# Two expert tiles of the first batch, routed during attention and run while the last batch is routed

## The chip, the cores and the metric

The kernel runs on one core of a Trainium2 chip. The metric is the time of one execution on the device in microseconds (us). The engines are named as the profile names them: PE is TensorE (PEld its weight loads), DVE is VectorE, ACT is ScalarE, POOL is GpSimd, SP is SyncE, whose queue issues most of the DMAs.

## What is computed

Three stages follow each other, cut here to what matters:

```python
def attention(q, k, v):                    # 4 batches, 8 heads, 768 rows, 64 wide
    scores = q @ k.T / 8                   # kept: the first 4 keys, and the last 128 up to the row
    return softmax(scores) @ v
x = attention(...)                         # as 3072 rows of 512
logits = x @ w_gate + modality_bias[modality_id]      # 8 experts
e = argmax(logits); gate = softmax(logits)[e]
moe[rows of e] = gate * (relu(x[rows] @ w1[e]) @ w2[e])   # w1 512x1024, w2 1024x512
h = moe @ w_in                             # 512x2048
out = (h * sigmoid(1.702 * h)) @ w_out     # 2048x512
```

Every row goes to one expert only. All of it is float32. The wide products are made from a rounded part (hi) and the rest (lo) of each operand as hi*hi + hi*lo + lo*hi in the type fp32r, so each operand is "split": one pass rounds it (ScalarE or GpSimd), another subtracts (VectorE or GpSimd).

## The kernel before

**Attention** goes over 4 batches of 8 heads of 6 row blocks (48 steps for a batch, `each_step`). At step n TensorE makes the scores of block n (lines 753, 754), turns the probabilities of block n-3 (line 765) and weighs the values of block n-4 (line 790). VectorE masks scores (line 1396), ScalarE makes the exponentials (line 1054) and copies turned probabilities out of PSUM (line 1079; VectorE does so for a head's last block, line 1408). All engines run their steps in program order, so what is put in a step holds up what stands behind it. After a head VectorE divides it by its row sums into `x_sb` (at step 4 of the next head). GpSimd splits q and k of the heads (lines 578 to 587); the arrays have four slots, so it may start head g only when head g-4's scores are made.

SyncE's queue works pair by pair (two heads, g from 0 to 15). For each pair it waits for `heads_done` of both heads, stores their part of x to DRAM (line 400), loads vT for pair g+3 (line 388), then v and q, k of the next batch (lines 377, 379, 372), and at last 256 KB of the second layer's input weights `w_in` into `win_raw` (line 395).

**Routing.** The logits of the heads are made inside attention. Batches 0 to 2 are routed during batch 3's attention (GpSimd and VectorE, `route_early`). The last batch is routed behind attention: argmax on VectorE, ranks by small matmuls (lines 864 to 870), positions, a sort of tokens into tiles of 128 rows by 24 one-hot matmuls (line 880), then the same for the gates (line 888). Between these, TensorE runs filler matmuls (`keep_going`, line 854). The first expert's weights are loaded (line 459, four pieces of 1 MB) when the ranks are known.

**The expert loop** takes a tile of 128 rows of one expert: GpSimd gathers rows by an indirect DMA (line 680), TensorE turns them (line 899), ScalarE rounds (line 1125), VectorE subtracts (line 1593), TensorE multiplies by w1 (lines 914 to 916, 24 matmuls), ScalarE applies relu (line 1132), TensorE turns the result (line 926) and multiplies by w2 (lines 939 to 941, 24 matmuls); VectorE scales by the gate (line 1608), GpSimd scatters the rows to `y_rows` (line 689). GpSimd splits `win_raw` among the first four tiles (lines 661, 663). The loop's length and each tile's expert are read from a table made by the routing. Then the dense second layer follows (lines 973 to 984).

Of the kernel before, what the change touches and what calls it, by code (L numbers as in the profile page):

```python
# [22 lines left out]
P = 128  # L23
BANK = 512
F32 = mybir.dt.float32
# [12 lines left out]
DMA = 16  # L38


def program(nc, qkT, vT, vP, modality, w_gate, bias, w1, w2, w_in, w_out, out, n_sink, window):
# [18 lines left out]
    EXP_AT, RANK_AT_STEP = 41, 41  # L60
    WARM_UP = 7
    CH = DM // P
# [4 lines left out]
    LEAD = 4  # L67
    YW = DM + 1
# [55 lines left out]
    with ExitStack() as ctx:  # L124
# [52 lines left out]
        q_st = place("q_st", [P, SLOT, S], F32R, at=ZW)  # L177
        k_hi = place("k_hi", [P, SLOT, KEYS], F32R)
        k_lo = place("k_lo", [P, SLOT, KEYS], F32R)
        v_sb = place("v_sb", [P, PAIRS, QT, VPAIR])  # L180
        x_sb = place("x_sb", [P, QT, DM])
        assert top[0] <= ZW + 2 * HALVES
        qk_raw = place("qk_raw", [P, SLOT, 2, S], at=ZS)
# [60 lines left out]
        table_f = place("table_f", [P, TAB])  # L244
        s_msk = place("s_msk", [P, RING, WMAX])
        assert top[0] <= ZS

# [3 lines left out]
        oh_slot = place("oh_slot", [P, NTILE, P], F32R, at=ZW + 2 * HALVES)  # L251
        tile_eq = place("tile_eq", [P, NTILE, SLOTS])
        tile_tok = place("tile_tok", [P, NTILE, SLOTS], F32R)
        assert top[0] <= ZW + 2 * HALVES + CH * F2
# [5 lines left out]
        GATES_AT = top[0]  # L260
# [3 lines left out]
        assert top[0] <= ZS  # L264
        tile_gate = place("tile_gate", [P, NTILE, 2, SLOTS], F32R, at=GATES_AT)
# [50 lines left out]
        expert_known, consts_copied = sem("expert_known"), sem("consts_copied")  # L316
        ohs_ready = sem("ohs_ready")
# [43 lines left out]
        TURN_AFTER = {5 + 2 * t: t for t in range(GT)}  # L361

# [4 lines left out]
        def _(sp):  # L367
# [55 lines left out]
            for h in range(SLOT + 1, H):  # L423

                sp.wait_ge(qk_split, 3 * (h - SLOT))
                load_qk(0, h)
                if h == SLOT + 1:
                    load_vt(2)
            for b in range(B):
                for c in range(PAIRS):  # L430
# [32 lines left out]
            load_win(B * PAIRS - 1)  # L463
            sp.wait_ge(runs_ready, 1)
            total = sp.value_load(table[0:1, TOTAL:TOTAL + 1], min_val=NTILE - 4, max_val=SLOTS - 4) + 4
# [13 lines left out]
            def rows_of(g):  # L479

                tiles = (g + 1) * GT + GT + E
# [33 lines left out]
        def _(pool):  # L515
# [74 lines left out]
            for h in range(1, B * H):  # L590
                split_qk(*divmod(h, SLOT))

            full, some = [P, NTILE, E], [P, PRE, E]
# [4 lines left out]
            pool.wait_ge(consts_loaded, 32)  # L598
            then(pool.tensor_copy(mod_f[:], mod_i[:, :, 0]))
            for m in range(NM):  # L600
                then(pool.tensor_scalar(mod_eq[:], mod_f[:], float(m), None, ALU.is_equal))
                to = bias_of[:] if m == 0 else biases[:]
                then(pool.tensor_tensor(to, col(mod_eq[:], full), bias_sb[:, m:m + 1, :].broadcast_to(full), ALU.mult))
                if m:
                    then(pool.tensor_tensor(bias_of[:], bias_of[:], biases[:], ALU.add))
            pool.wait_ge(logits_added, B - 1)
            pool.tensor_tensor(lg[:, 0:PRE, :], lg[:, 0:PRE, :], bias_of[:, 0:PRE, :], ALU.add).then_inc(pre_biased, 1)

            pool.wait_ge(best_found, 1)
# [6 lines left out]
                .then_inc(ties_marked, 1)  # L616

# [9 lines left out]
            then(pool.tensor_copy(acc[:, 1], hot[:, 0]))  # L627
            for t in range(1, QT - 1):
                then(pool.tensor_tensor(acc[:, t + 1], acc[:, t].bitcast(F32), hot[:, t], ALU.add))
# [10 lines left out]
            pool.wait_ge(rows_known, 1)  # L640
            for t in range(PRE):
                pool.tensor_scalar(oh_slot[:, t, :], iota_row[:], rank_p[:, t:t + 1], None, ALU.is_equal)\
                    .then_inc(rows_marked, 1)

# [1087 lines left out]
```

## Time and profile before

| | us |
|---|---|
| median of 3 runs | 1115.92 (1115.02 to 1116.5) |
| the profiled execution | 1115.81 |
| its span | 1113.9 |
| TensorE busy | 1101.5 (99%) |
| VectorE, ScalarE, GpSimd busy | 424.2, 378.1, 327.0 |
| mean granted TensorE clock | 0.997 of 2.4 GHz |

The span goes from the first to the last instruction of the profiled execution. A busy TensorE is one with matmuls in flight; they overlap, so starts matter more than durations. In the span attention takes about the first 234 us, the last batch's routing goes on to about 262, the expert loop to about 585 and the second layer to the end. A row in order of time gives the start and the duration in us, the engine, the line, the operation with its output and inputs, the shapes, how many were merged, and in brackets how long the engine had been idle before it and what ended that. A row of groups gives count, busy us, mean ns of one, and the idle time before.

### The profile page before, as it was taken

The numbers are of one execution on the slowest core, as the hardware profiler recorded it, in microseconds if no ns is written. First come the engines' busy times: TensorE is split into PE (matmuls) and PEld (weight loads), VectorE is DVE, ScalarE is ACT, GpSimd is POOL, SyncE is SP. The second block draws the span as 40 slices with busy tenths as digits, with TensorE's granted clock in tenths as the row PEclk, the third lists the DMA queues.
The fourth block names the chain that finished last, engine by engine and source line by source line (L and its number), as shares of the span: only waits on it lengthen the run. The fifth ranks groups of instructions, "written<-read, shape, count | busy, mean of one in ns | idle before, by whom it ended". The sixth has DMA issues, their size and how long they took to land.

```text
span 1113.9 us, 18738 instructions
## 1 busy us (share of the span) xinstructions
PE 1101.5 (99%) x5952; PEld 943.1 (85%) x5953; DVE 424.2 (38%) x1089; ACT 378.1 (34%) x781; POOL 327.0 (29%) x441
## 2 busy tenths in 40 slices
PE   9999999999999999999999999999999999999998
PEld 8999999987888888888888888888888888888887
DVE  5566666685121233221265323222322222222222
ACT  3666666643221233222253222222222222222222
POOL 8898888644642212121121001001001001000100
PEclk9999999989999999999999999999999999999999
DMA  9999988237111123211132101001000000000101
GB/s 222 234 259 243 229 223 222 73 124 264 38 47 47 41 99 139 79 47 38 38 125 103 29 1 48 19 9 38 28 9 38 19 19 28 9 0 0 39 1 38
DMA packets 57393, 92.04 MB, mean 83 GB/s; under 512 B 7937, under 2 KB 32769, under 8 KB 57345
## 3 DMA queue, kind: packets, MB, share of 16 engines
q1 hardware_dynamic: 51584, 72.56, 24.2%
q0 software_dynamic: 5760, 18.89, 4.9%
q8 instruction: 24, 0.39, 0.2%
q14 instruction: 25, 0.20, 0.1%
HBM read 72.02 MB, written 19.41 MB: 82 GB/s over the span
## 4 chain that ended last, share of the span: by engine, by line
PE 92%; DVE 3%; ACT 2%; issue 2%; POOL 1%; ACTq 0%; DVEq 0%; POOLq 0%
PE psum L982 8%; PE psum L984 8%; PE psum L983 8%; PE psum L975 8%; PE psum L973 8%; PE psum L974 8%; PE psum L790 5%; PE psum L939 4%; PE psum L914 4%; PE psum L941 4%; PE psum L916 4%; PE psum L915 4%; PE psum L940 4%; PE psum L765 2%; PE psum L926 2%; PE psum L753 2%
## 5 line engine op out<-in xcount | busy, mean ns | idle before, releaser
L1654 DVE TENSOR_TENSOR g<-psum,g 128x512 f32<-128x512 f32 x96 | 66.3, 691 | 292.3 <-ACT g L1178 292.3
L1178 ACT ACTIVATE g<-psum 128x512 f32<-128x512 f32 x96 | 57.3, 598 | 306.5 <-PE psum L975 305.7
L982 PE MATMUL psum<-w_hi,gT_hi 128*128 128x512 f32 x384 | 151.3, 394 | 0.0
L984 PE MATMUL psum<-w_hi,gT_lo 128*128 128x512 f32 x384 | 149.6, 390 | 0.0
L983 PE MATMUL psum<-w_lo,gT_hi 128*128 128x512 f32 x384 | 149.6, 389 | 0.0
L975 PE MATMUL psum<-x2T,win_lo 128*128 (+1 forms) x384 | 149.5, 389 | 0.0
L973 PE MATMUL psum<-x2T,win_hi 128*128 (+1 forms) x384 | 149.5, 389 | 0.0
L974 PE MATMUL psum<-x2T,win_hi 128*128 (+1 forms) x384 | 149.4, 389 | 0.0
L722 POOL DMA_INDIRECT out<-o_out,out_rows x20 | 21.5, 1075 | 406.6 <-ACT o_out L1198 402.0
L790 PE MATMUL psum<-v_sb,pT 128*128 128x73 f32 x704 | 106.0, 269 | 2.4 <-DVE pT L1408 1.2
L1396 DVE CUSTOM_DVE_ANT_0 s_msk<-psum,mask_sb 128x260 f32<-128x260 f32 (+1 forms) x192 | 75.0, 403 | 70.7 <-PE psum L754 37.5
L790 PEld LDWEIGHTS psum<-v_sb,pT 128*128 128x128 f32 x704 | 93.4, 191 | 8.9 <-DVE pT L1408 7.5
L1054 ACT ACTIVATE probs<-s_msk,negmax 128x260 f32<-128x260 f32 (+1 forms) x192 | 93.5, 494 | 13.8 <-DVE negmax L1396 13.6
L1661 DVE TENSOR_TENSOR gT_lo<-g,gT_hi 128x512 fp32r<-128x512 f32 x96 | 66.4, 693 | 64.5 <-ACT gT_hi L1185 64.5
L914 PE MATMUL psum<-w_hi,xsT_hi 128*128 128x512 f32 x208 | 83.3, 400 | 2.0 <-DVE xsT_lo L1593 2.0
L984 PEld LDWEIGHTS psum<-w_hi,gT_lo 128*128 128x128 f32 x384 | 72.1, 188 | 15.3
L975 PEld LDWEIGHTS psum<-x2T,win_lo 128*128 128x128 f32 x384 | 72.1, 188 | 15.0
L974 PEld LDWEIGHTS psum<-x2T,win_hi 128*128 128x128 f32 x384 | 72.1, 188 | 15.0
L1185 ACT CAST gT_hi<-g 128x512 fp32r<-128x512 f32 x96 | 59.6, 621 | 74.1 <-DVE g L1654 74.1
L973 PEld LDWEIGHTS psum<-x2T,win_hi 128*128 128x128 f32 x384 | 72.1, 188 | 14.9
L983 PEld LDWEIGHTS psum<-w_lo,gT_hi 128*128 128x128 f32 x384 | 72.2, 188 | 14.4
L982 PEld LDWEIGHTS psum<-w_hi,gT_hi 128*128 128x128 f32 x384 | 72.1, 188 | 14.3
(229 smaller groups left out, 1991.4 us busy)
## 6 DMA issues: line engine op xcount, KB each, us to landing
qk_raw<-qkT SPq DMA_DIRECT2D x64, 384.0 KB, 7.6
stage<-w SPq DMA_DIRECT2D x12, 1024.0 KB, 6.9
x<-y_rows SPq DMA_DIRECT2D x24, 256.5 KB, 2.6
vT_sb<-vT SPq DMA_DIRECT2D x16, 384.0 KB, 6.0
v_sb<-vP SPq DMA_DIRECT2D x16, 384.0 KB
x_rows<-x_sb SPq DMA_DIRECT2D x16, 384.0 KB, 3.2
win_raw<-w_in SPq DMA_DIRECT2D x16, 256.0 KB, 8.7
stage<-w_out SPq DMA_DIRECT2D x4, 1024.0 KB, 6.6
```

The costliest lines, as they stand in the source:

```text
L790: mm = pe.matmul(o, pT[:, n % 2, k * P:(k + 1) * P], v_sb[:, c, kb, half * VEXT:(half + 1) * VEXT], start=(i == 0 and k == 0), stop=(k == ...
L914: pe.matmul(psum[:, HB[hf], :], xsT_hi[:, c, :], hi, start=(c == 0), stop=False)
L973: pe.matmul(bank, wh, hi, start=(c == 0), stop=False)
L974: pe.matmul(bank, wh, lo, start=False, stop=False)
L975: mm = pe.matmul(bank, win_lo[:, c, f * P:(f + 1) * P], hi, start=False, stop=(c == CH - 1))
L982: pe.matmul(psum[:, OB[t], :], gh, hi, start=(f == 0), stop=False)
L983: pe.matmul(psum[:, OB[t], :], gh, lo, start=False, stop=False)
L984: return pe.matmul(psum[:, OB[t], :], gT_lo[:, f % 4, t * P:(t + 1) * P], hi, start=False, stop=(f == F2C - 1))
L1054: act.activation(probs[:, n % RING, 0:width[i]], s_msk[:, n % RING, 0:width[i]], ACT.Exp, bias=negmax[:, n % 8:n % 8 + 1], scale=-1.0).the ...
L1396: dve.tensor_tensor_reduce(s_msk[:, n % RING, 0:width[i]], psum[:, S_ps[n % 3], 0:width[i]], mask_sb[:, min(i, MASKS - 1), 0:width[i]], -S ...
L1654: dve.tensor_tensor(g32[:, f % 2, :], psum[:, FB[f % 2], :], g32[:, f % 2, :], ALU.mult)\
L1661: dve.tensor_tensor(gT_lo[:, f % 4, :], g32[:, f % 2, :], gT_hi[:, f % 4, :].bitcast(F32), ALU.subtract).then_inc(gT_split, 1)
```

## The change

Two tiles ("open" tiles, `OPEN = 2`) are filled with the first batch's rows of the expert that most of them choose, up to 256 rows.

- Batch 0 is routed by itself during batch 1: GpSimd makes logits, ties, one-hots and running counts between its head splits (`between`, behind heads 9, 11, 12, 13, 17, 18, 25), VectorE the reductions in steps 9 to 46 of batch 1, TensorE the ranks at step 29. In step 42 VectorE waits for GpSimd (`open_chosen`). In batch 2 a sort gives tokens and gates of the two tiles. The rows taken are subtracted from the expert's ranks, so that the loop does not hold them.
- SyncE loads that expert's w1 and w2 in 16 parts of 128x512 (256 KB), two with each pair from pair 7 to 14, behind the vT load and ahead of the next batch's v, q and k. The 16 loads of `w_in` leave attention and are issued when both open tiles are done.
- ScalarE rounds part j at step 2 of head 17+j (`round_open`), GpSimd subtracts it behind the split of head 21+j, the last four behind its one-hots.
- GpSimd gathers the open rows near the end of batch 3. TensorE turns the first tile in the tail of attention.
- Behind attention TensorE runs the two open tiles' matmuls with the routing's small matmuls in between, in an order written out by hand; the filler is gone. In `up` and `down` the products of a half are grouped: all hi*hi, then hi*lo, then lo*hi, each group with its own wait. `EXP_AT`, `RANK_AT_STEP` and the steps of `route_early` move back by 1 to 5.
- Arrays are placed anew: the open tiles use the room of `win_hi` and `win_raw`; `x_sb` lies where `w_hi` is later, so ScalarE waits for the last stores of x before it rounds the first run's weights.

```diff
@@ SyncE, for each pair
                     store_pair(b, c)
                     if g + 3 < B * PAIRS:
                         load_vt(g + 3)
+                    if g == OPEN_LOAD:
+                        sp.wait_ge(open_expert_known, 1)
+                        chosen = sp.value_load(open_e[0:1, 0:1], min_val=0, max_val=E - 1)
+                    if OPEN_LOAD <= g < OPEN_LOAD + OPEN_PARTS // 2:
+                        load_open(g - OPEN_LOAD, chosen)
...
-                    if g + 1 < B * PAIRS:
-                        load_win(g)
@@ SyncE, behind attention
-                        if q == 2:
-                            sp.wait_ge(gathered, 16)
...
-            load_win(B * PAIRS - 1)
+            sp.wait_ge(y_ready, OPEN)
+            for n in range(QUARTERS * PIECES):
+                load_win(n)
@@ GpSimd
+            between = {9: make_biases, 11: open_logits, 12: open_ties, 13: open_chain, 17: open_choice,
+                       18: open_marks, 25: open_rows}
             for h in range(1, B * H):
                 split_qk(*divmod(h, SLOT))
+                if h in between:
+                    between[h]()
+                if h >= OPEN_BACK:
+                    split_open(h - OPEN_BACK)
@@ ScalarE, in each step
+                if b == 1 and n == 2 * QT + 2:
+                    act.wait_ge(open_shifted, 1)
+                    act.activation(o_exps[:], o_below[:], ACT.Exp).then_inc(open_exped, 1)
+                j = (b * HT + n - 2) // QT - OPEN_HEAD
+                if n % QT == 2 and 0 <= j < OPEN_PARTS and (n < HT or b == B - 1):
...
+                    round_open(j)
...
+            def round_open(j):
+                q, cols = open_part(j)
+                act.wait_ge(open_loaded[j // 2], 32)
+                act.copy(win_hi[:, q, cols], win_raw[:, q, cols]).then_inc(open_high, 1)
@@ TensorE, behind attention (the filler calls keep_going go)
+            for hf, part in ((0, 0), (0, 1), (1, 0)):
+                up_open(0, hf, part)
+            rank_own()
+            turn_open(1)
+            up_open(0, 1, 1)
+            turn_h(0)
+            for hf in range(2):
+                for part in range(2):
+                    up_open(1, hf, part)
+            pe.wait_ge(heads_done, B * H + AHEAD)
+            down_open(0, 0, 0)
+            sort_tokens()
+            down_open(0, 0, 1)
+            down_open(0, 1, 0)
+            down_open(0, 1, 1)
+            turn_h(1)
             turn_xs(0)
+            sort_gates()
+            down_open(1, 0, 0)
+            down_open(1, 0, 1)
             up(0, 0)
             turn_xs(1)
+            down_open(1, 1, 0)
+            down_open(1, 1, 1)
@@ VectorE, in batch 1
+                if n == 42:
+                    dve.wait_ge(open_chosen, 1)
+                    then(dve.tensor_reduce(o_row[:], o_rank[:], AX.X, ALU.add))
+                if n == 43:
+                    then(dve.tensor_reduce(o_most[:], o_which[:], AX.X, ALU.add))
+                if n == 44:
+                    dve.tensor_copy(open_e[:], o_most[:]).then_inc(open_expert_known, 1)
```

## Rows read from the trace of the kernel before

**Rows 1.** Page, costliest groups: expert up part, first of three products.
```profile
L914 PE MATMUL psum<-w_hi,xsT_hi 128*128 128x512 f32 x208 | 83.3, 400 | 2.0 <-DVE xsT_lo L1593 2.0
```

**Rows 2.** Windows, attention and gap: busy PE, PEld, DVE, ACT, POOL; clock; DMA.
```profile
160.00:200.00 40.00, 39.48 (x327) 37.34 (x325) 25.32 (x120) 25.56 (x75) 32.46 (x37) 1.00 0.89 219
244.00:252.00 8.00, 8.00 (x44) 8.00 (x45) 6.82 (x16) 3.80 (x2) 1.24 (x1) 0.57 0.57 204
```

**Rows 3.** TensorE in order of time between attention and the expert loop.
```profile
233.25 0.71 PE L795 MATMUL psum<-v_sinks,pT_sinks 128*128 128x292 f32 x2
...
236.24 0.30 PE L864 MATMUL psum<-seen,ones 128*128 128x64 f32 x1 [0.51 <-DVE onehot L1324]
...
242.62 3.34 PE L880 MATMUL psum<-tile_tok,oh_slot 128*128 128x32 f32 x24 [1.20 <-DVE tile_tok L1498]
...
256.28 0.50 PE L914 MATMUL psum<-w_hi,xsT_hi 128*128 128x512 f32 x1 [1.47 <-DVE xsT_lo L1593]
...
261.87 0.60 PE L899 MATMUL psum<-ident,xs 128*128 128x128 f32 x4
262.58 1.09 PE L926 MATMUL psum<-ident,h 128*128 128x128 f32 x8
264.20 0.49 PE L914 MATMUL psum<-w_hi,xsT_hi 128*128 128x512 f32 x1 [0.53 <-DVE xsT_lo L1593]
```

**Rows 4.** TensorE in order of time, first up matmul of two following tiles.
```profile
276.46 0.47 PE L914 MATMUL psum<-w_hi,xsT_hi 128*128 128x512 f32 x1
...
288.76 0.48 PE L914 MATMUL psum<-w_hi,xsT_hi 128*128 128x512 f32 x1
```

**Rows 5.** SyncE's issues in order of time, pairs 8 and 12.
```profile
142.54 0.40 SPq L400 DMA_DIRECT2D x_rows<-x_sb  x1
142.98 0.54 SPq L388 DMA_DIRECT2D vT_sb<-vT  x1
...
197.00 0.40 SPq L400 DMA_DIRECT2D x_rows<-x_sb  x1
...
198.03 0.73 SPq L395 DMA_DIRECT2D win_raw<-w_in  x1
```

**Rows 6.** DMA issues of pairs 8, 12: KB each, us to landing.
```profile
vT_sb<-vT SPq DMA_DIRECT2D x1, 384.0 KB, 4.3
...
vT_sb<-vT SPq DMA_DIRECT2D x1, 384.0 KB, 5.4
win_raw<-w_in SPq DMA_DIRECT2D x1, 256.0 KB, 5.4
```

**Rows 7.** ScalarE in order of time, head 19, and one pass of 128x512.
```profile
143.81 0.81 ACT L1054 ACTIVATE probs<-s_msk,negmax 128x128 f32<-128x128 f32 x2
145.28 0.27 ACT L1079 COPY pT<-psum 128x128 f32<-128x128 f32 x1 [0.67 <-PE psum L765]
...
254.85 0.59 ACT L1125 CAST xsT_hi<-psum 128x512 fp32r<-128x512 f32 x1 [4.88 <-PE psum L899]
```

**Rows 8.** TensorE in order of time, value matmuls of head 19's first block.
```profile
146.88 0.34 PE L790 MATMUL psum<-v_sb,pT 128*128 128x73 f32 x2
```

**Rows 9.** GpSimd in order of time: splits of two heads, the bias block.
```profile
53.36 0.84 POOL L578 CAST q_st<-qk_raw 128x768 fp32r<-128x768 f32 x1
...
57.10 1.82 POOL L585 TENSOR_TENSOR k_lo<-qk_raw,k_hi 128x768 fp32r<-128x768 f32 x1
...
59.04 0.83 POOL L578 CAST q_st<-qk_raw 128x768 fp32r<-128x768 f32 x1
...
207.81 0.19 POOL L599 CAST mod_f<-mod_i 128x24 f32<-128x24 int32 x1
...
210.70 0.52 POOL L607 TENSOR_TENSOR lg<-lg,bias_of 128x144 f32<-128x144 f32 x1
```

**Rows 10.** VectorE in order of time around step 42 of batch 1.
```profile
115.25 0.28 DVE L1396 CUSTOM_DVE_ANT_0 s_msk<-psum,mask_sb 128x128 f32<-128x128 f32 x1
...
117.37 0.41 DVE L1408 COPY pT<-psum 128x256 f32<-128x256 f32 x1
```

More of the change, by code:

```diff
@@ L588, in split_qk, with col, row, make_biases @@
                     .then_inc(qk_split, 1)
+            full, some, batch = [P, NTILE, E], [P, PRE, E], [P, QT, E]
+            def col(v, shape):
+                return v.rearrange("p (t o) -> p t o", o=1).broadcast_to(shape)
+            def row(v, shape):
+                return v.rearrange("p (o e) -> p o e", o=1).broadcast_to(shape)
+            def make_biases():
+                pool.wait_ge(consts_loaded, 32)
+                then(pool.tensor_copy(mod_f[:], mod_i[:, :, 0]))
+                for m in range(NM):
+                    then(pool.tensor_scalar(mod_eq[:], mod_f[:], float(m), None, ALU.is_equal))
+                    to = bias_of[:] if m == 0 else biases[:]
+                    then(pool.tensor_tensor(to, col(mod_eq[:], full), bias_sb[:, m:m + 1, :].broadcast_to(full),
+                                            ALU.mult))
+                    if m:
+                        then(pool.tensor_tensor(bias_of[:], bias_of[:], biases[:], ALU.add))
@@ new lines, in open_logits, with open_ties @@
+            def open_logits():
+                pool.wait_ge(logits_added, 1)
+                pool.tensor_tensor(o_lg[:], lg[:, 0:QT, :], bias_of[:, 0:QT, :], ALU.add).then_inc(open_biased, 1)
+            def open_ties():
+                pool.wait_ge(open_best, 1)
+                pool.tensor_tensor(o_below[:], o_lg[:], col(o_best[:], batch), ALU.subtract).then_inc(open_shifted, 1)
+                pool.wait_ge(open_shifted, 1)
+                then(pool.tensor_scalar(o_tied[:], o_below[:], 0.0, None, ALU.is_equal))
+                pool.tensor_tensor(o_tied[:], o_tied[:], row(from_end[:], batch), ALU.mult).then_inc(open_tied, 1)
@@ new lines, in open_chain @@
+            def open_chain():
+                pool.wait_ge(open_lead, 1)
+                then(pool.tensor_tensor(o_tied[:], o_tied[:], col(o_lead[:], batch), ALU.subtract))
+                then(pool.tensor_scalar(o_hot[:], o_tied[:], 0.0, None, ALU.is_equal))
+                then(pool.tensor_scalar(o_seen[:, 0, :], from_end[:], 0.0, None, ALU.mult))
+                for t in range(QT):
+                    then(pool.tensor_tensor(o_seen[:, t + 1, :], o_seen[:, t, :].bitcast(F32),
+                                            o_hot[:, t, :].bitcast(F32), ALU.add))
+                pool.sem_inc(open_seen, 1)
@@ L626, in _ @@
             acc = seen[:, 0:PRE, :].rearrange("p (b t) e -> p t b e", b=B - 1)
-            then(pool.tensor_copy(acc[:, 1], hot[:, 0]))
-            for t in range(1, QT - 1):
+            for t in range(QT - 1):
                 then(pool.tensor_tensor(acc[:, t + 1], acc[:, t].bitcast(F32), hot[:, t], ALU.add))
@@ L643, in _ @@
                     .then_inc(rows_marked, 1)
+            for j in range(B * H - OPEN_BACK + 1, OPEN_PARTS):
+                split_open(j)
             def finish_scatter():
@@ L841, in step @@
                     weigh_values(b, n - PV_LAG)
+                if b == B - 1 and n == HT + 1:
+                    turn_open(0)
             def warm_up():
@@ new lines, in down_open @@
+            def down_open(t, hf, part):
+                chunks = [(hf * FC // 2 + k, slice(k * DM, (k + 1) * DM)) for k in range(FC // 2)]
+                if part == 0:
+                    pe.wait_ge(y_moved, t + PRIMED)
+                    pe.wait_ge(hT_high, t * 2 + hf + 1)
+                    pe.wait_ge(open_high, 4 * (hf + 3))
+                    for f, cols in chunks:
+                        pe.matmul(psum[:, YB, :], hT_hi[:, f, :], win_hi[:, 2 + hf, cols], start=(f == 0), stop=False)
+                else:
+                    pe.wait_ge(open_split, 4 * (hf + 3))
+                    for f, cols in chunks:
+                        pe.matmul(psum[:, YB, :], hT_hi[:, f, :], win_lo[:, 2 + hf, cols], start=False, stop=False)
+                    pe.wait_ge(hT_split, t * 2 + (hf + 1 + H_FREE))
+                    for f, cols in chunks:
+                        mm = pe.matmul(psum[:, YB, :], hT_lo[:, f, :], win_hi[:, 2 + hf, cols],
+                                       start=False, stop=(f == FC - 1))
+                    if hf:
+                        mm.then_inc(y_ready, 1)
@@ new lines, in up @@
+                    pe.wait_ge(w1_split, r * 2 + hf + 1)
+                    for c in range(CH):
+                        pe.matmul(psum[:, HB[hf], :], xsT_hi[:, c, :], w_lo[:, hf, chunks[c]], start=False, stop=False)
+                    if hf == 0:
+                        pe.wait_ge(xsT_split, t + 1 + PRIMED)
+                    for c in range(CH):
+                        mm = pe.matmul(psum[:, HB[hf], :], xsT_lo[:, c, :], w_hi[:, hf, chunks[c]],
+                                       start=False, stop=(c == CH - 1))
```

530 lines of the change are left out of this document (379 added, 151 removed).

## The prediction, made before any run of the change

> **What bounds the kernel now.** I read the page's costliest groups, then busy time by stage, then the engines in order of time where stages meet. The 208 matmuls at line 914, eight to a tile, say that 26 expert tiles run [rows 1]. In attention TensorE is busy 39.5 of 40 us at the full clock, while GpSimd is busy 32.5 and the DMA engines 0.89 of the time [rows 2]. So in attention a delay of TensorE is not won back, and GpSimd's spare time is small. The gain has to come from the stretch behind attention. The last attention matmul ends at about 233.9 us and the expert loop's first transpose starts at 262.58 [rows 3]: 28.7 us in which much of what TensorE does is filler (line 854, dropped by the change). A tile in the loop takes 12.30 us, from 276.46 to 288.76 [rows 4].
>
> **What is removed.** In those 28.7 us the useful work is: rank matmuls 1.1 us (236.24 to about 237.3), the two sorts of 24 matmuls at 3.34 (the tokens' stands in the rows, the gates' is as long), two groups of four transposes at 0.45 (the second from 261.87), and the first tile's up part from 256.28 to 261.87, 5.6; together 14.3 [rows 3]. The other 14.4 us are filler and waits. The change puts two tiles' work, 2 x 12.3 = 24.6 us, in front and between the sorts, and takes it from the loop: with the reference's seeded inputs the first batch sends 399 rows to expert 0, so both tiles are full, and the experts' counts 1567, 1497 and 8 (13 + 12 + 1 = 26 tiles, as the trace has it) become 11 + 12 + 1. So the loop starts at 233.9 + 14.3 + 24.6 = 272.8 if TensorE never waits, and has two tiles fewer: 24.6 - (272.8 - 262.6) = 14.4 us won. The stall of 0.7 us in the old loop's first pass (transposes from 262.58 for 0.87, next matmul at 264.20 [rows 3]) goes too, as the split of the second gathered tile is done by then. Against it, the transposes of tile 0's second half are late: its relu can only start when the eight matmuls behind the ranks end, and with 0.59 us for such a ScalarE pass [rows 7] TensorE waits some 0.5 us. Net **-14.6**. Between 13 and 15.5: the token sort now ends near 252 and not 246, so the first gather is issued near 253.5 and wanted near 257.3, where it may be a microsecond late.
>
> **What is costed at nothing.** Grouping the hi and lo products of a tile leaves their number and size alone. The run weights (4 MB) still come at the routing's end, but are now wanted at 264 us, not at 256. The second layer's input weights leave attention and load after both open tiles, hidden by 24 loop tiles. On GpSimd a head's split takes 5.68 us [rows 9] of TensorE's 6.8 per head; from head 21 on each also carries the split of a 128x512 part, two thirds of the 1.82 that 768 elements take [rows 9], so 1.2: 6.9 in all. It no longer gains on TensorE, but it doesn't collapse, as it may run 15 us behind (it works three heads ahead) and I count 8. If that cover went, every microsecond beyond would be TensorE's.
>
> **A wait of VectorE, step 42 of batch 1.** It waits there for GpSimd's choice. GpSimd, which starts head 9's split at 59.04 [rows 9], then does the bias block (207.81 to 210.70, 2.9 us, moved here [rows 9]), eight heads at 5.68, and 17 small operations at about 0.3, so it is done at 59.0 + 5.7 + 2.9 + 45.4 + 5.3 = 118.3. VectorE is at the wait at 115.6 (mask at 115.25 [rows 10]). Queued behind it is the copy of turned probabilities at 117.37 [rows 10], and it comes 2.9 late; I give TensorE 0.4 of slack before it wants the copy. **+2.5**, between 0 (GpSimd on time) and 4.
>
> **A wait of ScalarE, eight times.** This term decides. SyncE issues part pair k of the expert's weights (2 x 256 KB) behind the store of x and the load of vT of pair 7+k, and that store waits for step 4 of head 16+2k. ScalarE rounds the first of them at step 2 of head 17+2k, four steps later, in order, with the exponentials and copies of probabilities queued behind. Take T as the store's issue, 142.54 for pair 8, 0.44 ahead of vT's [rows 5]. ScalarE ends the exponential before that place at 144.62, T+2.1; the next copy is at 145.28 [rows 7]; TensorE starts the matmuls on it at 146.88, T+4.34 [rows 8]. When do the parts land? The vT load, issued at 142.98, landed 4.3 us later, T+4.7 [rows 5, 6], and the parts are behind it. With pair 12, vT (issued 0.45 behind its store, too) landed at T+5.9 and one more piece of 256 KB, issued at 198.03, 5.4 later, T+6.4 [rows 5, 6]. So a piece adds 0.6, or 1.1 by what the full DMA engines move in attention (219 GB/s at 0.89 [rows 2]). Two pieces give T+5.9 to 6.9 from pair 8, T+7.0 to 7.5 from pair 12; I take T+6.7. Then 0.59 for rounding, 0.27 for the copy and 0.15 of handing over: TensorE goes on at T+7.7, **3.4 us late**. The next store is tied to TensorE's progress, so this comes again with each pair. Six pairs have vT ahead; the last two don't, some 1.3 us less to move. 6 x 3.4 + 2 x 2.1 = **+24.6** (with L for the landing after T, some 8L - 29.3). Below, parts landing with vT at T+4.8, it is 9; above, at T+7.5, 31. The odd parts are there already and their 0.6 us fit into ScalarE's waits.
>
> The Trainium skill ("DMA: Bandwidth & Descriptors", Anatomy of one DMA) gives about 2 us fixed and 436 GB/s behind it. By that, an estimate, the 1.31 MB of a pair would be there 5.0 us after T, ahead of what these rows show, and the term would be 11 us instead of 24.6.
>
> **Sum.** -14.6 + 2.5 + 24.6 = +12.5, so 1115.8 + 12.5 = **1128** us, against the profiled execution's own 1115.81 (span 1113.9), which is 0.1 below the median of the three runs, 1115.92. About 0.2% (2.2 us) is what a measurement of this kernel can tell from no change.
>
> **Rivals.**
> 1. *The parts are there in time.* The gain stands: 1115.8 - 14.6 + 2.5 = 1103.7. It needs a landing before about T+3.3. At T+5.2 loss and gain are equal. For it: the queue is nearly empty at T, since the earlier pairs' input weights have left it. Against: vT alone takes to T+4.7. Chance with its neighbourhood below T+4.9: 0.19.
> 2. *Landing near T+5.1*: 8 x 5.1 - 29.3 = 11.5 of loss, no change, 1115. Rows for it are vT's T+4.7 with pieces that add 0.2 each; this is the case that the page's rate gives. 0.06.
> 3. *The clock falls as well.* In the gap TensorE idled 1.2 us before the tokens' sort and then ran small matmuls; the grant fell to 0.57 on average over 244 to 252 [rows 2, 3], its lower level (1.2 GHz) for most of it, which takes 0.43 x 8 = 3.4 us of work away. A wait of over 3 us in each pair may do that again: eight falls add 27, 1155; four, 1142. For: the waits are longer than that one. Against: full clock in all of attention, dense work between them. 0.20. The Trainium skill ("TensorE: Matmul & The Clock Gate", HAM oscillation) describes just such a cycle, each wait for a DMA followed by work at the low clock.
> 4. *It doesn't do what it says*: the open tiles not full, one tile more, +12.3 to 1140. The counts exclude it but for a fault: 0.01.
>
> The forecast itself, waits on the parts with the clock held, 1117 to 1138, has 0.54. Faster 0.20, same 0.05, slower 0.75. The range reaches from rival 1 to half of rival 3: 1102 to 1145.
>
> **What would show it.** Right: in attention, idle time of ScalarE before a copy of win_hi (the even parts), released by the DMA, 4 to 5 us eight times; TensorE idle before the value matmuls of row block 0 of heads 17, 19, to 31, about 3 us each; attention ending near 261, first expert matmul right behind it, the loop 24 tiles long, 39 us after attention's end; VectorE waiting about 3 us once near 116. Wrong: parts that land within 3.3 us, TensorE without idle time in attention, or a granted clock below 1 in attention.

## The result, and the profile after

| | before | after |
|---|---|---|
| median | 1115.61 (4 runs) | 1161.97 (4 runs, 1160.31 to 1172.69) |
| ratio | | 1.0435, 95% interval 1.0372 to 1.0498 |
| span of the profiled execution | 1113.9 | 1158.5 |
| mean granted TensorE clock | 0.997 | 0.972 |
| attention's last matmul ends | 233.96 [rows 3] | 283.04 |
| first dense matmul starts | 572.63 | 617.86 |

The kernel is 46 us slower, not 12. The change does what it says: 24 loop tiles and two open ones. TensorE's groups and waits over the whole span, of the kernel after:

```profile
L964 PE MATMUL psum<-v_sb,pT 128*128 128x73 f32 x704 | 115.3, 287 | 21.3 <-ACT pT L1355 15.4 <-DVE pT L1772 4.7 <-issue 0.2
L1158 PE MATMUL psum<-w_hi,xsT_hi 128*128 128x512 f32 x192 | 53.7, 401 | 0.0
...
ACT win_hi L1383 <- DMA win_raw<-w: 27.5, 8, 4.7
```

192 matmuls at line 1158 are 24 tiles, against the 26 of [rows 1]. TensorE was idle for 2.4 us in all ahead of the value matmuls before; now (line 964) it is 21.3, of which 15.4, in seven waits, for ScalarE's copy. ScalarE itself waits eight times, 27.5 us, for the expert's weight parts. Pair 7, by SyncE, ScalarE and TensorE in order of time (SPq is SyncE's queue), answers to [rows 5, 7, 8]:

```profile
134.14 0.40 SPq L458 DMA_DIRECT2D x_rows<-x_sb  x1
134.59 0.54 SPq L446 DMA_DIRECT2D vT_sb<-vT  x1
136.72 0.88 SPq L495 DMA_DIRECT2D win_raw<-w  x2
...
136.58 0.80 ACT L1330 ACTIVATE probs<-s_msk,negmax 128x128 f32<-128x128 f32 x2
141.55 0.62 ACT L1383 CAST win_hi<-win_raw 128x512 fp32r<-128x512 f32 x1 [4.17 <-DMA win_raw<-w]
142.07 0.26 ACT L1355 COPY pT<-psum 128x128 f32<-128x128 f32 x1
...
142.38 0.44 PE L964 MATMUL psum<-v_sb,pT 128*128 128x73 f32 x2 [3.18 <-ACT pT L1355]
...
143.17 0.56 PE L964 MATMUL psum<-v_sb,pT 128*128 128x73 f32 x4
...
144.20 0.97 PE L964 MATMUL psum<-v_sb,pT 128*128 128x73 f32 x4
```

The store is T, 134.14. The copy stands in ScalarE's queue behind the rounding, and TensorE waits 3.18 us for it. The last two rows show something else: four value matmuls take 0.56 us right behind the wait and 0.97 one microsecond later. The windows of the kernel after (busy PE, PEld, DVE, ACT, POOL; granted clock; DMA share; GB/s) say why:

```profile
120.00:140.00 20.00, 16.97 (x120) 15.68 (x120) 12.00 (x58) 9.21 (x26) 18.70 (x33) 0.91 0.67 164
140.00:160.00 20.00, 17.50 (x109) 16.95 (x109) 7.58 (x36) 9.47 (x27) 13.94 (x15) 0.74 0.56 143
160.00:180.00 20.00, 17.88 (x98) 17.22 (x98) 8.79 (x38) 8.63 (x25) 11.85 (x14) 0.66 0.56 140
180.00:200.00 20.00, 18.23 (x99) 17.33 (x99) 7.38 (x36) 8.21 (x24) 12.96 (x16) 0.66 0.59 151
200.00:220.00 20.00, 16.62 (x126) 15.73 (x124) 9.52 (x43) 10.31 (x29) 14.96 (x18) 0.91 0.67 167
220.00:240.00 20.00, 17.30 (x135) 15.55 (x133) 11.35 (x55) 11.23 (x32) 17.39 (x18) 1.00 0.82 228
240.00:260.00 20.00, 18.25 (x110) 17.38 (x110) 8.20 (x41) 9.54 (x27) 9.50 (x10) 0.74 0.16 50
...
144.00:148.00 4.00, 4.00 (x21) 4.00 (x21) 0.74 (x4) 1.81 (x7) 3.84 (x5) 0.50 1.00 223
148.00:152.00 4.00, 4.00 (x21) 4.00 (x21) 1.06 (x4) 1.11 (x4) 2.25 (x3) 0.50 0.11 23
```

[Rows 2] had 1.00 throughout attention. Now the clock is at its lower level (0.50, 1.2 GHz) from 144 to 152, and the busy shares of TensorE don't show it: from 180 to 200 it is "busy" 18.23 of 20 us and makes 99 matmuls, where [rows 2] had 327 in 40 us: 60% of the work. 20 us times what is missing to 1.00 in the seven long rows, 1.38, is 27.6 us of lost work. The low clock comes in six stretches. One stands behind a wait of 2.88 us at 122 us (VectorE's at step 42 of batch 1, below), the other five at five of the seven waits for ScalarE. How long a wait was does not sort them: at the one of 1.65 us (ended at 185.07) the clock fell, behind the one of 1.84 us (ended at 225.86) it did not, and it stands at 1.00 from 220 to 240.

Behind attention the forecast gain of 14.6 us shrank to 338.7 - 334.8 = 3.9 (from the last attention matmul to the first dense one). TensorE in order of time, then VectorE with GpSimd beside it, then the third gather's issue:

```profile
296.17 1.20 PE L1079 MATMUL psum<-win_hi,xsT_lo 128*128 128x512 f32 x4 [3.08 <-DVE xsT_lo L1840]
...
325.10 1.03 PE L1177 MATMUL psum<-ident,h 128*128 128x128 f32 x8
...
337.43 1.11 PE L1049 MATMUL psum<-ident,xs 128*128 128x128 f32 x4 [5.83 <-DMA xs<-x_rows,gather_i]
...
290.81 4.58 DVE L1878 TENSOR_TENSOR pos_t<-pos_t,rank_t 128x24 f32<-128x24 f32 x1
...
290.38 4.97 POOL L741 TENSOR_TENSOR win_lo<-win_raw,win_hi 128x512 fp32r<-128x512 f32 x4
...
329.99 1.05 POOL L843 DMA_INDIRECT xs<-x_rows,gather_i  x1 [0.82 <-POOL scatter_i L820]
...
325.29 8.62 SPq L453 DMA_DIRECT2D win_raw<-w_in  x16
337.12 4.46 SPq L528 DMA_DIRECT2D stage<-w  x4
```

An addition of 24 elements took 4.58 us and ended with GpSimd's four splits (290.38 + 4.97 = 295.35, against 295.39). And the third gather was issued 4.7 us after the first of the 16 loads of `w_in`, in the midst of them (their issues run from 325.29 to 333.91).

### The profile page after: what moved, and what is told of

Its sections match the earlier page's. It is cut to its first block, busy times and chain, and to the rows that moved or that the text cites. A ratio compares the mean times of both kernels' runs of the same rounds, so it can differ in the third digit from the quotient of the medians.

```text
span 1158.5 us, 18600 instructions
## 1 busy us (share of the span) xinstructions
PE 1120.7 (97%) x5883; PEld 960.0 (83%) x5884; DVE 434.6 (38%) x1109; ACT 385.2 (33%) x798; POOL 354.5 (31%) x492
## 4 chain that ended last, share of the span: by engine, by line
PE 84%; POOL 6%; DVE 3%; DMA 3%; issue 2%; SPq 1%; ACT 1%; POOLq 0%; DVEq 0%; ACTq 0%
PE psum L1258 8%; PE psum L1259 8%; PE psum L1260 8%; PE psum L1251 8%; PE psum L1250 8%; PE psum L1249 8%; PE psum L1189 4%; PE psum L1192 4%; PE psum L1195 4%; PE psum L964 4%; PE psum L1158 3%; PE psum L1162 3%; PE psum L1166 3%; DMA win_raw<-w 2%; PE psum L1177 2%
## 5 line engine op out<-in xcount | busy, mean ns | idle before, releaser
L964 PE MATMUL psum<-v_sb,pT 128*128 128x73 f32 x704 | 115.3, 287 | 21.3 <-ACT pT L1355 15.4
L964 PEld LDWEIGHTS psum<-v_sb,pT 128*128 128x128 f32 x704 | 103.9, 210 | 28.9 <-ACT pT L1355 17.1
L1355 ACT COPY pT<-psum 128x256 f32<-128x256 f32 (+1 forms) x160 | 55.8, 349 | 83.4 <-PE psum L939 80.8
```

Source lines behind the costliest of these rows:

```text
L964: mm = pe.matmul(o, pT[:, n % 2, k * P:(k + 1) * P], v_sb[:, c, kb, half * VEXT:(half + 1) * VEXT], start=(i == 0 and k == 0), stop=(k == ...
```

## The experiments

All against one table, read from each kernel's profiled execution: where attention's last matmul ends, the time from there to the first dense matmul, and what TensorE lost between 100 us and attention's end, idle and by the clock ((1 - granted clock) times the time). The profiled execution is one of several: that of the kernel with four edits is the fastest of its 12, 4.7 us under its median, so its row looks better than that kernel is.

| kernel | median | att. ends | behind | idle | clock |
|---|---|---|---|---|---|
| before | 1115.6 | 234.0 | 338.7 | 1.1 | 0 |
| after | 1162.0 | 283.0 | 334.8 | 21.2 | 27.3 |
| rounded one head later | 1121.0 | 242.6 | 335.1 | 6.9 | 0 |
| 20 fillers | 1155.6 | 276.8 | 336.3 | 4.9 | 0 |
| 9 fillers | 1149.9 | 269.6 | 336.8 | 11.6 | 6.8 |
| parts issued first | 1125.6 | 249.0 | 335.7 | 9.2 | 3.4 |
| gather first | 1162.0 | 284.3 | 333.3 | 20.0 | 30.7 |
| splits early | 1160.5 | 287.4 | 331.9 | 21.1 | 33.3 |
| behind-attention edits alone | 1158.7 | 287.0 | 328.6 | 21.5 | 32.4 |
| later and paced | 1116.4 | 241.4 | 333.0 | 4.5 | 0 |
| four edits | 1115.5 | 242.3 | 326.1 | 5.7 | 0.2 |
| five edits | 1115.1 | 244.0 | 328.5 | 5.5 | 2.4 |
| routing first | 1111.0 | 242.4 | 327.0 | 4.3 | 1.8 |
| tail in order | 1110.4 | 238.7 | 329.4 | 2.2 | 0 |

Theory: the parts come late, and each wait is paid twice, as itself and in the low clock behind it. Rivals: the clock falls for another reason, or costs little.

**The parts rounded one head later.**

```diff
-    OPEN, OPEN_LOAD, OPEN_HEAD = 2, 7, 17
+    OPEN, OPEN_LOAD, OPEN_HEAD = 2, 7, 18
...
+            round_open(OPEN_PARTS - 1)
             relu_half(0, 0)
```

> The changed kernel, with ScalarE rounding each weight part one head later (part j at step 2 of head 18+j, the last one behind the attention steps), 6.8 us after the place where it waited up to 4.7 us. Theory (the waits for the parts cost TensorE 15.4 us, and the low clock behind each of them 27 us in all): both go, no idle time of ScalarE before win_hi, the clock at 1.00 from 140 to 280 us, attention ends near 241 us, time near 1120. Rival (the low clock comes from other loads in attention, not from these waits): 15 us less, near 1147, clock still at 0.5 in stretches.

1120.96 (1116.47 to 1122.42), ratio 1.0041, interval 1.0019 to 1.0064: as expected, 41 us back. ScalarE's waits for the parts are gone; the clock, in the windows of this kernel:

```profile
120.00:160.00 40.00, 36.74 (x298) 34.60 (x299) 26.54 (x120) 24.41 (x69) 38.23 (x54) 1.00 0.84 215
160.00:200.00 40.00, 39.48 (x327) 37.33 (x326) 24.97 (x116) 28.67 (x81) 38.77 (x43) 1.00 0.92 241
```

From 160 to 200 TensorE is busy 39.48 us with 327 matmuls, as in [rows 2], beside all the added work of the other engines. So the parts' lateness is what attention lost, and GpSimd's splits cost it nothing there.

**Filler in the waits.** The same waits, but TensorE kept busy; 20 float32 matmuls of 128 columns ahead of the value matmuls of heads 17, 19, to 31:

```diff
+                if n < HT and (b * HT + n - PV_LAG) % (2 * QT) == QT and b * HT + n - PV_LAG >= 17 * QT:
+                    pe.wait_ge(heads_done, b * H + ((n - PV_LAG) // QT - 1 + AHEAD))
+                    for _ in range(20):
+                        pe.matmul(psum[:, O_ps[1], 0:P], ident[:], ident[:], start=True, stop=True)
```

> The changed kernel with its waits kept, and 20 filler matmuls (128 columns, 2.4 us at the full clock) on TensorE ahead of the value matmuls that wait for the parts, eight times. They compute nothing. Theory (the clock falls because TensorE is idle in the wait): the idle time is filled, the clock stays up in most of the eight stretches, and up to 27 us come back: 1135 to 1145. Rival (the clock falls for another reason, or a filled wait does not count): the clock falls as before, time 1162 or up to 10 us more, as the filler outlasts the shorter waits at the low clock.

1155.63 (1154.87 to 1162.72), ratio 1.0373, interval 1.0344 to 1.0402. That is above the 1135 to 1145 expected: a group took 4.6 us, double what I had reckoned (each such matmul stands in the trace as two records), so 37 us of filler hide the effect in the time. But ScalarE waits as before (30.9 us, 8 times) and in attention the clock never falls, in the windows of this kernel:

```profile
120.00:160.00 40.00, 36.71 (x304) 34.77 (x304) 22.73 (x103) 19.47 (x56) 36.91 (x54) 1.00 0.73 191
160.00:200.00 40.00, 39.76 (x341) 38.48 (x340) 17.99 (x85) 21.47 (x61) 29.52 (x34) 1.00 0.77 180
```

So it falls for TensorE's idle time and not for the late loads themselves. Not every idle stretch does it, though: the wait at step 42 is 2.96 us in the kernel rounded later and 2.88 here, with a clock of 1.00 behind it in both, where the kernel after, with the same 2.88 us, had a fall. With half the filler:

```diff
-                    for _ in range(20):
+                    for _ in range(9):
```

> The kernel after, with 9 instead of 20 filler matmuls (2.1 us by the 4.6 us that 20 took) on TensorE ahead of the value matmuls that wait for the rounding. They fall in the waits of 1.4 to 3.3 us and so cost 0 to 4 us in all. Theory: the waits themselves (15 us) stay, the clock holds at 1.00 through attention, and the 27 us of low clock are gone: 1134 to 1142. Rival: the time goes with the waits alone, and the clock's fall costs little: 1155 to 1165.

1149.87 (1141.46 to 1152.02), ratio 1.0293, interval 1.0260 to 1.0326. This missed its range: the clock fell a little still, 6.8 us. Against the kernel after, attention ends 13.5 us sooner: 20.5 less lost to the clock, 9.6 less idle, 8 x 2.1 = 17 of filler added. That account closes (20.5 + 9.6 - 17 = 13), so the low clock cost its own 20 us in time, not only in the windows. The rival (the clock costs little, 1155 to 1165) is out. The kernel after shows it by itself: its four executions, of 1160.3, 1161.3, 1162.6 and 1172.7 us, had a mean granted clock of 0.972, 0.969, 0.968 and 0.964.

**The parts issued ahead of store and vT.**

```diff
                     sp.wait_ge(heads_done, b * H + (2 * c + 2 + AHEAD))
-                    store_pair(b, c)
-                    if g + 3 < B * PAIRS:
-                        load_vt(g + 3)
                     if g == OPEN_LOAD:
...
                         load_open(g - OPEN_LOAD, chosen)
+                    store_pair(b, c)
+                    if g + 3 < B * PAIRS:
+                        load_vt(g + 3)
```

> The kernel after, with only SP's order within a pair changed: the two weight parts issued ahead of the store of x and of the load of vT. Theory: the parts land some 2 us sooner after the pair's end (about T+4 to T+5.5 instead of T+6 to T+7.4), since they are issued 0.9 us sooner and nothing of this pair is ahead of them in the queues; ScalarE's wait of 3.4 us on average falls to 1 to 2 us, TensorE's waits ahead of the value matmuls from 15.4 to under 4 us, the clock falls go as well, and the time is 1120 to 1132. Rival: the loads land late because of all that is in flight, whatever the order, or vT comes late in their place: 1145 to 1162.

1125.60 (1122.69 to 1127.20), ratio 1.0082, interval 1.0068 to 1.0097, as expected. TensorE's waits for ScalarE's copy fall from 15.4 to 2.9 us. The rounding of pair 8's parts, in ScalarE's order of time, and the parts' landing (KB each, us) of this kernel, against 4.1 us in the kernel after:

```profile
154.85 0.62 ACT L1383 CAST win_hi<-win_raw 128x512 fp32r<-128x512 f32 x1 [1.46 <-DMA win_raw<-w]
...
win_raw<-w SPq DMA_DIRECT2D x16, 256.0 KB, 2.9
```

36 us from the order of three issues in a queue: the store and vT ahead of the parts are what made them late.

**Behind attention.** Three edits to the kernel after, the first two alone. The third gather ahead of the ten operations that make the scatter's indices:

```diff
             gather(1)
-            finish_scatter()
             gather(2)
+            finish_scatter()
```

> The changed kernel with one line moved on GpSimd: the third gather goes out ahead of the scatter table's ten operations, as in the kernel before. Theory (that gather is issued at 330.0 us, 7.8 us after its buffer is free, and then sits behind 4 MB of w_in in the DMA queues, so TensorE idles 5.8 us and runs some 5 us at the low clock): TensorE no longer waits at the third turn of rows, 5.8 us and about 2.5 us of clock come back, near 1154. Rival (the DMA queues are the cause, full of w_in from 325 us): the wait only shrinks by a microsecond or two, or moves to the next gather.

1162.01 (1158.41 to 1170.35), ratio 1.0427, interval 1.0386 to 1.0467: nothing, where 1154 was expected. The third gather's wait is gone and only moved, to the next gather, which GpSimd issues behind the open scatter's landing (GpSimd, then TensorE, of this kernel):

```profile
341.29 0.19 POOL L839 COPY gather_col<-gather_i 128x1 int32<-128x1 int32 x1 [8.05 <-DMA y_rows<-open_ys,open_scatter]
...
349.58 1.12 PE L1049 MATMUL psum<-ident,xs 128*128 128x128 f32 x4 [6.13 <-DMA xs<-x_rows,gather_col]
```

Three of GpSimd's last splits ahead of its one-hots:

```diff
+            for j in range(B * H - OPEN_BACK + 1, OPEN_PARTS - 1):
+                split_open(j)
             pool.wait_ge(rows_known, 1)
...
-            for j in range(B * H - OPEN_BACK + 1, OPEN_PARTS):
-                split_open(j)
+            split_open(OPEN_PARTS - 1)
```

> The changed kernel with GpSimd subtracting weight parts 12, 13 and 14 ahead of its one-hots of rows, and only part 15 behind them. Theory (VectorE's 24-element addition at line 1878 took 4.58 us because it was held until GpSimd's four subtractions of 128x512 ended, and TensorE then waited 3.1 us for the low part of the second open tile): the addition takes at most 1.5 us, the 3.1 us are gone and the low clock behind them (297 to 301 us): 3 to 5 us less, near 1158. Rival (VectorE is held by something else, such as a wait of its own): the addition still takes over 4 us.

1160.46 (1156.56 to 1163.17), ratio 1.0399, interval 1.0375 to 1.0424. The addition of 24 elements, in VectorE's order of time:

```profile
296.77 0.18 DVE L1879 TENSOR_TENSOR pos_t<-pos_t,rank_t 128x24 f32<-128x24 f32 x1
```

0.18 us for 4.58, and the wait for the low part (line 1079 in the kernel after) is gone. The time behind attention is 2.9 us shorter (331.9); in the median that drowns in what the clock does.

**The loads paced**, on the kernel rounded later: one quarter of `w_in` for each finished tile, and a quarter of the second expert behind it, for 8 MB in one go.

```diff
             sp.wait_ge(y_ready, OPEN)
-            for n in range(QUARTERS * PIECES):
+            for n in range(PIECES):
                 load_win(n)
             sp.wait_ge(runs_ready, 1)
...
+            for q in range(QUARTERS):
+                sp.wait_ge(y_ready, OPEN + 1 + q)
+                if q + 1 < QUARTERS:
+                    for n in range((q + 1) * PIECES, (q + 2) * PIECES):
+                        load_win(n)
+                load_run(1, second, (q,))
...
```

> The rounded-later kernel (1121.0 us) with the pacing alone: one quarter of w_in per finished tile, the second expert's loads behind it at the same pace. Theory: the full DMA queues are why the third gather came 6.2 us late, so this wait goes to under 1.5 us, with the 1 to 3 us of low clock behind it: 1111 to 1116. The 3.1 us wait for xsT_lo stays. Rival: the gather is late because it is issued behind GpSimd's ten operations of the scatter indices, not because of the queues: the wait stays at 4 to 6 us and the time at 1119 to 1122.

1116.38 (1113.04 to 1119.31), ratio 1.0006, interval 0.9996 to 1.0016, just above the 1111 to 1116 expected. The third gather is issued behind the indices as before; the transposes that wait for it, in TensorE's order of time, first without the pacing:

```profile
297.39 1.12 PE L1049 MATMUL psum<-ident,xs 128*128 128x128 f32 x4 [6.16 <-DMA xs<-x_rows,gather_i]
```

and with it, GpSimd's issue ahead:

```profile
289.49 1.05 POOL L850 DMA_INDIRECT xs<-x_rows,gather_i  x1 [0.82 <-POOL scatter_i L827]
...
292.82 0.66 PE L1056 MATMUL psum<-ident,xs 128*128 128x128 f32 x4 [1.73 <-DMA xs<-x_rows,gather_i]
```

3.3 us after its issue TensorE has the rows, where it took 7.8 without the pacing (289.62 to 297.39) and 7.4 in the kernel after (329.99 to 337.43). So 4.4 us of the 6.2 were the full queues; the 1.73 left, more than the 1.5 expected, are the rival's share, the late issue (with the gather ahead as well, in the kernel with four edits, TensorE has no wait there). All three edits above on the kernel after, with the parts still late:

> The kernel after with the three edits behind attention alone (third gather ahead of the indices, three splits ahead of the one-hots, paced loads), and the weight parts rounded as in the kernel after. Theory: what is lost in attention (49 us) and behind it (10 of the forecast 14.6 us) adds up: attention ends at 282 to 287 as before, the stretch behind it to the dense layer's first matmul is 325 to 328 us instead of 334.8, and the time is 1151 to 1155. Rival: the losses behind attention are made up elsewhere and the pacing brings nothing once attention is late: 1158 to 1164.

1158.72 (1155.78 to 1163.18), ratio 1.0394, interval 1.0369 to 1.0418: above its range and in the rival's, though the stretch behind attention is 328.6, 6.2 shorter and just above the 325 to 328 expected. Attention took most of it: the clock lost 32.4 us there, not 27.3. That is no effect of the edits that I can show: the four executions of the kernel after, among which the profiled one is the fastest, differ in the clock by more.

**All together, and a version that beats both.** Rounding later, gather first, pacing, and all of GpSimd's splits ahead of its one-hots:

```diff
+            for j in range(B * H - OPEN_BACK + 1, OPEN_PARTS):
+                split_open(j)
             pool.wait_ge(rows_known, 1)
```

> Four edits together: every weight part rounded one head later (the run with 1121.0 us), the third gather issued ahead of the scatter's indices, all of GpSimd's splits ahead of its one-hots, and the 16 w_in loads paced: one quarter per finished tile from the second open tile on, with the second expert's loads behind them at the same pace instead of 8 MB at once. Theory: of the waits left in the rounded-later kernel, 3.1 us for xsT_lo (VectorE's addition held by GpSimd) and 6.2 us for the gather (full DMA queues) go, and with them the clock of 0.93 and 0.87 in 240 to 260 and 280 to 300; 1121.0 less 9 to 14 us is 1107 to 1112. Rival: the pacing only moves the collision into the loop (a wait for win_raw on GpSimd, or for the second expert's stage on ScalarE, of 5 us or more): 1112 to 1121.

1115.53 (1110.82 to 1119.78, 12 runs), ratio 1.0003, interval 0.9991 to 1.0015: above the 1107 to 1112 expected, and spread wide; the profiled execution, at 1110.8, is the fastest. The time follows the clock: the fastest had a mean of 0.998, the two above 1119 us 0.989 and 0.992. With VectorE's wait for `o_rank` moved (steps 42 to 46 become 47 to 51):

```diff
-                if n == 42:
+                if n == 47:
                     dve.wait_ge(open_chosen, 1)
...
```

> The same four edits and VectorE's five operations at steps 42 to 46 of the second batch (wait for GpSimd's o_rank first) moved to steps 47 to 51. Theory: VectorE no longer waits 3 us for o_rank, so TensorE's 2.9 us at 122 go: 3 us below the kernel with the four edits, 1104 to 1109. Rival: the expert then comes too late for SP, whose queue waits behind the store of pair 7, and the first weight part comes later: no gain, or a ScalarE wait for win_raw at 150.

1115.13 (1112.48 to 1119.03), ratio 1.0003, interval 0.9993 to 1.0014: no gain either, where 1104 to 1109 was expected. The wait at 122 is gone, but attention still ends 10 us later than before. TensorE near its end, and what GpSimd ended just ahead of the first row, in this kernel:

```profile
231.26 0.30 PE L1005 MATMUL psum<-onehot,tri 128*128 128x144 f32 x1 [2.78 <-issue]
...
242.11 0.79 PE L971 MATMUL psum<-v_sb,pT 128*128 128x73 f32 x4 [1.92 <-DVE pT L1780]
...
230.92 0.19 POOL L803 CAST seen<-batch_sum 128x8 fp32r<-128x8 f32 x1
```

The first waits for GpSimd's running sums (done at 231.11; the view names no releaser), and GpSimd did two splits and two gathers ahead of the first three batches' routing. So those go behind it:

```diff
-            split_open(B * H - OPEN_BACK)
             pool.wait_ge(best_found, 1)
...
-            gather_open()
...
             pool.sem_inc(tiles_seen, 1)
+            gather_open()
+            for j in range(B * H - OPEN_BACK, OPEN_PARTS - 2):
+                split_open(j)
...
```

> The kernel with all five edits (1115.1 us), and on GpSimd the two gathers of the open rows and the split of the twelfth part moved from ahead of the routing of the first three batches to behind it, the last two parts' splits behind four of the one-hots. In that kernel's profile TensorE waits 2.8 us at 231 for GpSimd's running sums, the clock is 0.57 from 232 to 236, and VectorE's bias addition at 240.1 takes 1.27 us beside the splits, with 1.9 us of TensorE's idle behind it. Theory: the routing ends 4 us sooner, the wait and the fall go, attention ends 3 to 5 us sooner, at 239 to 241 instead of 244, and the time is 1108 to 1112. Rival: VectorE, which has some 6 us of routing work for the last two heads whatever GpSimd does, sets attention's end: 0 to 1.5 us of gain, 1113 to 1116; or the open rows' gather comes late for its transposes and TensorE waits there.

1111.00 (1109.47 to 1113.88), ratio 0.9962, interval 0.9949 to 0.9975: 0.4% faster than before, small but clear of the interval. The theory got the time and not the way: attention ended at 242.4, since VectorE was held again, in its order of time with GpSimd's splits:

```profile
236.35 1.43 DVE L1664 TENSOR_SCALAR rank_t<-rank_cnt 128x18 f32<-128x18 f32 x1
...
234.00 3.73 POOL L748 TENSOR_TENSOR win_lo<-win_raw,win_hi 128x512 fp32r<-128x512 f32 x3
```

Last, VectorE's four operations behind the last copy of probabilities, and the last three splits one by one:

```diff
-                if t == 3:
-                    for j in range(OPEN_PARTS - 2, OPEN_PARTS):
-                        split_open(j)
+                if t in (1, 5, 9):
+                    split_open(OPEN_PARTS - 3 + t // 4)
...
-                if n == HT + 1:
+                if n == HT + 2:
                     add_heads(B - 1, H - 1)
```

> The kernel of 1111.0 us, with two orders changed at the end of attention: VectorE's four operations for the last batch's logits and ranks (1.3 us) moved from ahead of the last copy of probabilities to behind it, and GpSimd's last three splits one by one between one-hots instead of in rows of three and two. In that kernel's profile VectorE's 128x18 operation at 236.35 took 1.43 us and ended with GpSimd's splits, TensorE then waited 2.1 us at 240.2 for the copy, and the clock was 0.50 from 240 to 244. Theory: the wait falls under 0.5 us, attention ends at 239 to 240 instead of 242.4, the fall goes, and the time is 1106 to 1109. Rival: the moved operations come back as a wait for the last head's routing or for openT_lo: 1110 to 1112.

1110.40 (1109.43 to 1113.51), ratio 0.9958, interval 0.9944 to 0.9971: not to be told from 1111.0, and above the 1106 to 1109 expected. Attention ends at 238.7, a little sooner than expected, but 2.4 us come back behind it, the rival's case. VectorE, then GpSimd, of this kernel:

```profile
237.59 1.21 DVE L1757 TENSOR_TENSOR rank_t<-rank_t,own_rank 128x6 f32<-128x6 f32 x1
...
241.16 1.25 DVE L1618 TENSOR_TENSOR lg<-lg,lg_parts 128x48 f32<-128x48 f32 x1
...
244.76 1.18 DVE L1648 TENSOR_SCALAR expsum<-expsum 128x6 f32<-128x6 f32 x1
...
237.51 1.27 POOL L748 TENSOR_TENSOR win_lo<-win_raw,win_hi 128x512 fp32r<-128x512 f32 x1
...
241.06 1.28 POOL L748 TENSOR_TENSOR win_lo<-win_raw,win_hi 128x512 fp32r<-128x512 f32 x1
...
244.62 1.28 POOL L748 TENSOR_TENSOR win_lo<-win_raw,win_hi 128x512 fp32r<-128x512 f32 x1
```

Three operations on 6 to 48 elements take 1.2 us each, every one ending within 0.1 us of a split's end. Split by split, the holding is shared out and not avoided.

## Why the prediction was wrong

It had the direction and the place of the waits, held the clock to be safe, and missed its range, 1102 to 1145, by 17 us.

- **The clock** is the step that failed: the forecast was "waits on the parts with the clock held" (0.54), on the ground of dense work between the waits. It did not hold. Rival 3 priced it (27 us for eight falls); the loss was 27.3 us, in six stretches at the lower level, 3 to 14 us long, so 4.6 us for a fall and not the 3.4 taken from the gap of before. That eight at 3.4 and six at 4.6 come to the same is luck. [Rows 2, 3] already had such a fall behind an idle of 1.2 us, and the waits forecast were three times as long: rival 3 deserved the larger chance. The Trainium skill ("TensorE: Matmul & The Clock Gate", HAM oscillation) describes waits for a DMA, each followed by work at the low clock; the trace agrees in kind, with a fall at five of the seven waits for ScalarE.
- **ScalarE's waits** were right in place and cause, and the term too large: ScalarE waited eight times at the places named, released by the DMA, but TensorE was idle only seven times, 15.4 us in all, where the term was 24.6. The rounding started at T+7.4 in pair 7, T+6.3 in pair 8, T+6.4 on average over six pairs (T+6.7 taken), and T+5.1 and T+4.5 in the last two (5.4 taken). With these eight times less the term's own 3.3 us each the sum is 21.5, so the landing was nearly right. The other 6 us: TensorE came to the copy at T+4.5 to T+5.3 and not at T+4.3 (why, no run shows), went on 0.8 us after the rounding began and not 1.0, and lost nothing in the eighth wait. The rate of the Trainium skill ("DMA: Bandwidth & Descriptors", Anatomy of one DMA) gave T+5.0, an estimate; for the six the measurement is 0.6 to 2.4 us above it. The page fits that rate to single DMAs from GpSimd's queue, and these were four of SyncE's behind each other.
- **VectorE's wait at step 42** came as forecast: 2.88 us of VectorE, 2.88 of TensorE (+2.5), and a fall of the clock worth 1.7 us that was not in the term. VectorE, then TensorE, of the kernel after:

```profile
119.77 0.20 DVE L1701 TENSOR_REDUCE o_row<-o_rank 128x6 f32<-128x48 f32 x1 [2.88 <-POOL o_rank L711]
...
121.95 0.67 PE L964 MATMUL psum<-v_sb,pT 128*128 128x73 f32 x4 [2.88 <-DVE pT L1772]
```

  That it is on the path did not show: taking it away, beside four other edits, changed 1115.5 to 1115.1, but there TensorE waited only 1.0 us for it.
- **-14.6 behind attention** came out as -3.9. The tile count, the order and the sorts were right: with the edits the stretch was 12.6 us shorter (326.1) in the fastest execution of the kernel with four edits, and 11.7 (327.0) in that of 1111.0 us. Two things costed at nothing took 9 us and a fall of the clock behind each: GpSimd's splits, which I had weighed against TensorE alone, held VectorE (3.1 us); and `w_in`'s loads, "hidden by 24 loop tiles", kept the third gather waiting (5.8 us) in the same DMA queues. That the gather "may be a microsecond late" was said of the first one; it was the third that was late.

The account of the kernel after, first dense matmul to first dense matmul: 20.1 us of idle (15.4 for ScalarE, 2.9 at step 42, the rest in small waits), 27.3 of clock and a rest of 1.7 in attention (added work and small waits before 100 us, as I take it), less 3.9 behind it, is 45.2, which is 617.86 - 572.63.

What stays open: the kernel with four edits spreads over 9 us from run to run where the kernel before spreads over 2. The runs show that its slower executions have the lower mean clock, and the profiles that the same wait at step 42 is followed by a fall in some kernels and not in others. What decides it no run here shows.

## What to carry to other kernels

Price a wait of TensorE twice, as idle time and as the low clock that may follow it, unless something dense runs in it; a table of idle and clock loss by stage tells the two apart. Before a small load is moved behind a store and a larger load in one queue, look at what order alone does: here it was worth 36 us. And work that is "hidden" on GpSimd or in the DMA queues is to be checked against each user of the same resource, not against TensorE's pace alone.

## What was not expected of the hardware

- GpSimd's subtraction of two tensors in SBUF (128x512, 1.25 us) can hold a VectorE operation on SBUF, even of 24 elements; four of them in a row held it to the end of the fourth (4.58 us), and the other way round VectorE's 128x2048 subtraction (2.29 us) held two of GpSimd's 32-element operations at 2.39 and 2.42 us, where their like took 0.3 (kernel after, VectorE and GpSimd in order of time):

```profile
323.80 2.29 DVE L1994 TENSOR_TENSOR w_lo<-stage,w_hi 128x2048 fp32r<-128x2048 f32 x1
...
326.66 2.29 DVE L1994 TENSOR_TENSOR w_lo<-stage,w_hi 128x2048 fp32r<-128x2048 f32 x1
...
323.93 2.39 POOL L818 TENSOR_SCALAR tokens<-tokens,iota_dump 128x32 f32<-128x32 f32 x1
...
326.76 2.42 POOL L820 TENSOR_SCALAR scatter_i<-tokens,iota_dump 128x32 int32<-128x32 f32 x1
```

  Not every operation was held: VectorE's reduction to 128x24 just ahead of the held addition, beside the first split, took its usual 0.35 us. And GpSimd's one-hots (one tensor as input, 10.5 us in all) held nobody: VectorE's operations on 48 elements with two inputs in SBUF took 0.21 to 0.35 us beside them (283.75 to 285.54 in the kernel after). The Trainium skill ("SBUF — State Buffer", SBUF: two separate sides) has this as an exclusive lock of a shared pair of ports for the whole instruction. The traces agree for the subtractions, and add that VectorE did not get its turn between GpSimd's queued instructions; for the one-hots, which the page's wording would have hold an operation with two inputs in SBUF too, they do not, and the measurement decides.
- An indirect gather of 128 rows, issued among 4 MB of loads, reached TensorE after 7.4 us (kernel after) and 7.8 us (rounded one head later), and after 3.3 us with 1 MB issued ahead of it.
- A float32 matmul of 128 columns stands in the trace as two records, and 20 of them took 4.6 us at the full clock.
